# Where an attention kernel multiplies by the values: six key chunks at once in every second group, or three in each

## What is computed

```python
q_bits = (np.einsum('bhsd,dk->bhsk', q, proj) > 0)      # 6 bits a row; the same for k
mask = q_bucket[:, :, :, None] == k_bucket[:, :, None, :]
scores = np.where(mask, scale * (q @ k.T), -1e9)
attn = exp(scores - max); attn = attn / (sum(attn) + 1e-9)
out = attn @ v                                          # 2 x 8 heads, 768 rows, 64 wide
h = np.maximum(np.maximum(x @ w1, x @ w2), x @ w3); y = h @ w_out
u = y @ w_in; result = (u * sigmoid(1.702 * u)) @ w_out2
```

## Time and profile before

| | before |
|---|---|
| median of 3 runs | 671.94 us (671.91 to 671.98) |
| span of the profiled execution | 670.8 us |
| PE busy | 663.7 us, 99% |
| DVE busy | 495.9 us, 74% |
| ACT busy | 346.6 us, 52% |
| POOL busy | 474.2 us, 71% |

### The profile page before, as it was taken

One profiled execution on the slowest core, in us unless ns is written; L12 is line 12 of the kernel. 1 busy time (PEld: TensorE's weight loads), 2 busy tenths in 40 slices (PEclk: granted clock), 3 DMA queues, 4 the chain that ended last, 5 costly groups with the idle time before them and its releaser, 6 DMA issues.

```text
span 670.8 us, 11966 instructions
## 1 busy us (share of the span) xinstructions
PE 663.7 (99%) x3892; PEld 576.8 (86%) x3892; DVE 495.9 (74%) x976; ACT 346.6 (52%) x761; POOL 474.2 (71%) x538
## 2 busy tenths in 40 slices
PE   8999999999999999999999999999999999999998
PEld 6776777777777699999999999988898988989896
DVE  6878878788788799869778963678877666555554
ACT  6887777877777630011103453555545554454433
POOL 6774756788876899968870528799987776777710
PEclk9999999999999999999999999999999999999999
DMA  6673836638352111111110201212232124212102
GB/s 159 152 161 102 192 88 155 151 88 187 91 132 75 34 32 32 32 32 33 32 40 25 95 1 33 79 48 80 79 93 64 64 78 143 64 64 65 45 18 94
DMA packets 58492, 54.17 MB, mean 81 GB/s; under 512 B 28640, under 2 KB 47488, under 8 KB 58432
## 3 DMA queue, kind: packets, MB, share of 16 engines
q1 hardware_dynamic: 56784, 53.02, 29.2%
q10 hardware_dynamic: 1648, 0.39, 0.3%
HBM read 32.51 MB, written 3.15 MB: 53 GB/s over the span
## 4 chain that ended last, share of the span: by engine, by line
PE 88%; POOL 6%; issue 2%; ACT 1%; DVE 1%; DMA 1%; DVEq 0%; ACTq 0%; POOLq 0%
PE psO L1544 10%; PE psS L1522 10%; PE psR L1530 9%; PE psR L1628 7%; PE psR L1627 7%; PE psR L1629 7%; PE psS L1627 6%; PE psS L1628 6%; PE psS L1629 6%; PE psS L1730 4%; PE psS L1729 4%; PE psS L1728 4%; POOL w_lo L736 3%; PE psR L1470 1%; POOL w_raw L727 1%
## 5 line engine op out<-in xcount | busy, mean ns | idle before, releaser
L577 POOL TENSOR_SCALAR probs<-probs,lone,inv 128x768 f32<-128x768 f32 x96 | 93.9, 985 | 58.6 <-DVE inv L1145 58.5
L736 POOL TENSOR_TENSOR w_lo<-w_raw,w_hi 128x256 fp32r<-128x256 f32 x96 | 79.2, 838 | 44.6 <-ACT w_hi L982 43.9
L1128 DVE TENSOR_REDUCE neg_max<-psS 128x1 f32<-128x768 f32 x96 | 91.2, 950 | 12.9 <-PE psS L1522 8.7
L803 ACT ACTIVATE probs<-psS,neg_max 128x768 f32<-128x768 f32 x96 | 86.5, 901 | 15.7 <-DVE neg_max L1128 15.6
L560 POOL TENSOR_SCALAR w_hi<-w_raw 128x256 fp32r<-128x256 f32 (+1 forms) x79 | 49.0, 624 | 50.2 <-PE psS L1629 28.9
L812 ACT ACTIVATE probs_t<-psR 128x384 f32<-128x384 f32 x131 | 60.7, 491 | 31.2 <-PE psR L1530 30.7
L1530 PE MATMUL psR<-ident,probs 128*128 128x128 f32 x576 | 74.6, 273 | 0.4 <-POOL probs L577 0.2
L1530 PEld LDWEIGHTS psR<-ident,probs 128*128 128x128 f32 x576 | 66.5, 140 | 5.5 <-POOL probs L577 2.1
L1544 PE MATMUL psO<-probs_t,v_raw 128*64 128x384 f32 x384 | 68.8, 494 | 0.0
L1379 DVE TENSOR_TENSOR v_raw<-psR,early 128x384 f32<-128x384 f32 x64 | 35.3, 552 | 32.4 <-PE psR L1629 32.2
L1384 DVE TENSOR_TENSOR v_raw<-v_raw,bits 128x384 f32<-128x384 f32 x64 | 53.7, 841 | 6.7 <-ACT bits L1005 4.3
(11 more groups left out here) (275 smaller groups left out, 1881.5 us busy)
## 6 DMA issues: line engine op xcount, KB each, us to landing
w_raw<-in_moe_w_in SPq DMA_DIRECT2D x16, 512.0 KB, 3.4
w_raw<-in_moe_w_out SPq DMA_DIRECT2D x32, 256.0 KB, 2.7
w_raw<-in_moe_w SPq DMA_DIRECT2D x9, 512.0 KB, 3.8
h_lo<-w_hi SPq DMA_DIRECT2D x22, 192.0 KB, 3.3
h_hi<-w_hi SPq DMA_DIRECT2D x18, 192.0 KB, 3.4
w_raw<-in_q SPq DMA_DIRECT2D x16, 192.0 KB, 3.6
v_raw<-in_v SPq DMA_DIRECT2D x16, 192.0 KB, 2.5
stacks<-w_hi SPq DMA_DIRECT2D x16, 192.0 KB, 3.3
```

The lines of the kernel that those rows point to most:

```text
L577: pool.tensor_scalar(probs[i % PROBS][:, :], probs[i % PROBS][:, :], lone[:, i % 6:i % 6 + 1], inv[:, i % 6:i % 6 + 1], ALU.add, ALU.mult) ...
L736: pool.tensor_tensor(in2_slot(w_lo, n, which), in2_raw(n, PARTS2[which]), f32(in2_slot(w_hi, n, which)), ALU.subtract).then_inc(in2_split, 1)
L803: act.activation(probs[i % PROBS][:, :].rearrange("p (a b) -> p a b", a=2), psS[i % 2][:, :, 0:HALF], ACT.Exp, bias=neg_max[:, i % 6:i % 6 ...
L1128: dve.tensor_reduce(neg_max[:, i % 6:i % 6 + 1], psS[i % 2][:, :, 0:HALF], AX.XY, ALU.min).then_inc(max_ready, 1)
```

## The change

`times_values` of a unit now stands in one piece. In odd groups n (from 5) PE does all six chunks of unit (n-3)//2, where it did the first three; in even groups it does none, where it did the last three of the unit begun in the group before. In the written-out part, unit 0 has all its six chunks where it had three, and group 4 has none. The instructions are the same in kind and number, and so are the waits; ACT, DVE, POOL and SP keep their order.

```diff
             turn_probs(6, 0)
             turn_probs(6, 1)
-            for c in range(TH):
+            for c in range(NT):
                 times_values(0, c)
             turn_probs(7, 0)
...
                 if n < GROUPS:
                     scores(3 * n + 1)
-                u, part = (n - 3) // 2, (n - 3) % 2
-                for c in range(TH * part, TH * part + TH):
-                    times_values(u, c)
+                if n % 2 == 1:
+                    for c in range(NT):
+                        times_values((n - 3) // 2, c)
                 if st < 2 and p + 1 < PAIRS:
                     turn_qk(2 * p + 2 + st)
```

## The result

The changed kernel takes 697.4 us (median; 696.9 to 697.6), the kernel before 672.0 us (median of 4 runs). The ratio is 1.0376, with a 95% interval of 1.0361 to 1.0391: 3.8% slower. Forecast were 696.1 us and a range of 691 to 701.5.

What follows compares the result with a forecast made beforehand. PE was taken to set the pace, with the other engines' chain about as long as a group. 1.93 + 6 x 1.63 + 6 x 1.61 + 2 x 1.79 - 0.8 = 24.2 us on 671.94 gave 696.1 us, range 691 to 701.5.

Steps and rivals of the forecast that it cites:

- six chunks in one piece against three: Values burst ahead of group 4 and in odd groups 5 to 31: 4.09 us against 2.16, 1.93 more each.
- turn_qk: odd group starts: After even groups 4, 8, ... 24, PE waits for copy_qk; next group starts at 6.64 us instead of 6.95.
- last pair: scores, transposes, scores, burst: Groups 28 and 30, without turn_qk or project: PE's start times in us, with transposes waiting for POOL's norm; 0.14 saved.
- loss in the three kinds of pairs: Net us added per even and odd group: 1.63 with turn_qk, 1.61 with project, 1.79 with neither.
- the end: Group 32 without a burst: the last tile's norm sets the first product, which starts 0.8 us earlier after the last scores.
- ahead of group 4: Unit 0's longer burst in the written-out part adds 1.93 us with no cover, since PE hardly waits there.
- The hole and what ends it: In even groups PE stands still until copy_qk, make_bits or norm releases it; only 0.31, 0.32 or 0.14 us saved.
- The switching: Each of 15 values bursts that disappear takes 0.24 us of switching with it, but inside PE's even-group wait.
- The others keep up: Rival: DVE, ACT and POOL finish even groups in PE's 4.8 us; 3.6 us gained, 668.3 us; chance 3%.
- Nothing is refilled: Rival: even groups save nothing, or the wait grows as a late copy delays the next scores; 700 to 703 us; 11%.
- the clock falls: Rival: PE's stops in even groups drop its clock to 1.2 GHz for 14 bursts, 4 us more each; 750 us; 2%.
- What would show it: Signs in the changed profile: 4.09 us bursts, even groups about 6.6 us with PE stops, PE busy falling 1 to 2 us per pair.

## Why the prediction was right

The range held the time, the forecast was 1.3 us under it, and its steps can be read off one by one. Of the 1.3 us, 0.7 are no step of the working. The forecast added 1.1 us to a span to get a time. In every run for which both are on record the time is 1.76 to 1.86 us over the span, so the 670.8 us of the profile belong to a run that took some 0.7 us more than the median. From span to span the change cost 24.7 us, where 24.2 were worked out.

| step | worked out | measured |
|---|---|---|
| six chunks in one piece against three | +1.93 | 4.02 to 4.03 between starts against 2.08 to 2.09 |
| turn_qk: odd group starts | 6.64 | 6.67 |
| turn_qk: its burst starts | 9.20 | 9.23 |
| project: last half tile starts | 6.13 | 6.26 |
| project: burst starts | 9.38 | 9.43 |
| last pair: scores, transposes, scores, burst | 4.99, 6.6, 7.90, 8.77 | 4.98, 6.63, 7.90, 8.78 |
| loss in the three kinds of pairs | 1.63, 1.61, 1.79 | 1.68, 1.67, 1.82 |
| the end | -0.8 | -0.97 |
| ahead of group 4 | +1.93 | +2.22 |

- *What bounds the kernel.* Right: shortening DVE's chain is worth nothing in the kernel before.
- *The hole and what ends it.* Right in all three kinds of groups, releasers included. Each of the twelve pairs with other work beside it lost some 0.05 us more than worked out, 0.6 us together, which the end (0.17 more saved) and a feed-forward part 0.3 us shorter partly offset. One term was too small: from the end of the releaser to PE's start I had taken 0.06 us and bounded it by 0.09, from DVE to POOL. Behind make_bits it is 0.14 (180.52 to 180.66), and behind both halves of copy_qk in group 24 it is 0.14 as well.
- *Ahead of group 4.* 0.29 of the 2.22 had arisen before unit 0's burst, which started at 29.88 in place of 29.59. In the profiles of the other kernels, which are alike up to there, it starts between 29.4 and 30.1.
- *The switching.* Cutting a burst measures an entry and an exit at 0.33 us, where I had read 0.24. The changed kernel has 15 of them fewer and is slower: what it saves there lies in the hole. The Trainium skill, TensorEngine Tiling (Array Packing), Key Properties, says that a change of the tiling mode drains the engine. The 0.33 us agree with that; that they are a drain, and nothing else at the change, no run here shows.
- *The rivals.* "The others keep up" had its deciding point at copy_qk ending before 3.9 us. It ended at 5.8, as before. "Nothing is refilled" (700 us) and "the clock falls" (granted clock 1.00 throughout) did not happen.
- *What would show it.* Two details were told wrongly there. With project PE stops before the third half tile, not the second (the working had it right). And PE's busy time did not fall by 1 to 2 us per pair of groups: it rose, from 13.90 us in groups 20 and 21 to 14.08 in groups 24 and 25, and from 663.7 to 668.6 in all. What fell is its share, since each pair is longer by the stop.

What stays open is small: why an entry and an exit cost 0.33 us and not the 0.24 read from the rows, and what moves the start of unit 0's burst by some tenths from one profile to the next.

## What to carry to other kernels

On in-order engines a full bound engine can be in balance with a chain that is hidden under it; work that is moved from one period to the next is then paid where it arrives and not given back where it leaves. Before a step is moved, list for the place that it leaves what the next instructions wait for, and when these things are ready counted from the period's own start: the latest of them is the floor of that period. And at the place where it arrives, look not only for what it waits, but for what the other engines have queued behind the steps that it now delays.

## What the runs showed that was not expected

- Idle matmuls in a hole are free to within the measurement: 252 of them, 14 us of PE's time, changed the time by 0.2 us.
- A row maximum of 128x768 from the score buffer takes 950 ns and of 128x384 556 ns: half of the columns save 0.39 us and not half of the time.
- Cutting a burst that uses half of the output columns by six transposes costs 0.33 us.
- From the end of the copy that reads a bank (ACT's copy_qk, DVE's make_bits) to PE's next transposes into it are 0.14 us. In the kernel with the cut burst it is the same twice: copy_qk's halves end at 40.89 and 41.36, and the half tiles behind them start at 41.03 and 41.50.
